# The sums over blocks of V in a fused attention kernel: loaded together, and partly added on VectorE

## The reference, cut to what matters

```python
k_sum = k.reshape(B, H, nb, block, D).max(axis=3)
v_sum = v.reshape(B, H, nb, block, D).mean(axis=3)
scores_l = where(|i - j| < 16, scale * q @ k.T, -1e9)      # a window around each position
scores_s = scale * q @ k_sum.T + log(block)                # 24 block summaries
a = softmax(concat(scores_l, scores_s))
attn = a @ concat(v, v_sum)
h = x @ w_in; solu = h * softmax(h); x = layernorm(solu) * g_ln @ w_out
out = elu(x @ w2_in) @ w2_out
```

## Time and profile before

| | |
|---|---|
| median of 3 runs | 502.55 us (502.33 to 504.12) |
| the profiled execution's own time | 502.94 us |
| its span in the profile | 501.2 us |
| granted clock, mean over the span | 0.999 |

### The profile page before, as it was taken

The page is one execution under the profiler, slowest core; times in us unless marked ns, Lnnn a source line. Parts: engine busy times, 40 slices in busy tenths (PEclk is TensorE's granted clock), DMA queues, the critical chain, the costliest instruction groups (busy, mean ns, idle before and its releaser), DMA issues.

```text
span 501.2 us, 8050 instructions
## 1 busy us (share of the span) xinstructions
PE 489.5 (98%) x3042; PEld 405.6 (81%) x3042; DVE 237.1 (47%) x634; ACT 213.5 (43%) x439; POOL 132.8 (27%) x131
## 2 busy tenths in 40 slices
PE   8889999999999999999999999999999999999997
PEld 7656666787988988999888888888888888888885
DVE  3578787278535535533655554333323323323331
ACT  3678887067525535545544343132122213212212
POOL 3995899801020020133645442000000000000000
PEclk9999999999999999999999999999999999999999
DMA  9999993700000000720000000020000002000002
GB/s 198 207 209 225 221 266 128 321 1 0 2 0 1 0 1 1 258 80 0 1 0 1 0 1 1 0 85 0 1 0 1 0 0 84 0 0 0 0 0 84
DMA packets 41669, 29.81 MB, mean 59 GB/s; under 512 B 33452, under 2 KB 35500, under 8 KB 40620
## 3 DMA queue, kind: packets, MB, share of 16 engines
q1 hardware_dynamic: 41636, 29.37, 22.8%
HBM read 26.21 MB, written 3.15 MB: 59 GB/s over the span
## 4 chain that ended last, share of the span: by engine, by line
PE 85%; DVE 5%; SPq 4%; DMA 2%; ACT 2%; issue 2%; POOL 1%; DVEq 0%
PE bank L951 12%; PE bank L953 12%; PE bank L952 12%; PE bank L1181 9%; PE bank L1179 9%; PE bank L1180 9%; PE bank L1133 4%; PE bank L1135 4%; PE bank L1134 4%; PE bank L1039 3%; PE bank L1010 2%; PE bank L960 2%; PE bank L1119 2%; DMA qraw<-in_q 2%; PE bank L1019 2%
## 5 line engine op out<-in xcount | busy, mean ns | idle before, releaser
L702 ACT ACTIVATE ex<-bank 128x512 f32<-128x512 f32 x48 | 28.7, 598 | 127.9 <-PE bank L953 127.9
L929 DVE TENSOR_SCALAR ex<-ex 128x512 f32<-128x512 f32 x48 | 21.6, 449 | 116.5 <-ACT ex L702 116.5
L953 PE MATMUL bank<-yt_lo,w2in_hi 128*128 (+1 forms) x192 | 74.8, 389 | 0.0
L952 PE MATMUL bank<-yt_hi,w2in_lo 128*128 (+1 forms) x192 | 74.8, 389 | 0.0
L1179 PE MATMUL bank<-w2out_hi,g_hi 128*128 128x512 f32 x192 | 74.8, 389 | 0.0
L1181 PE MATMUL bank<-w2out_hi,g_lo 128*128 128x512 f32 x192 | 74.7, 389 | 0.0
L951 PE MATMUL bank<-yt_hi,w2in_hi 128*128 (+1 forms) x192 | 74.7, 389 | 0.0
L1180 PE MATMUL bank<-w2out_lo,g_hi 128*128 128x512 f32 x192 | 74.7, 389 | 0.0
L934 DVE TENSOR_TENSOR g_lo<-gf,g_hi 128x512 fp32r<-128x512 f32 x48 | 46.5, 969 | 35.9 <-ACT g_hi L710 35.9
L710 ACT ACTIVATE g_hi<-gf 128x512 fp32r<-128x512 f32 x48 | 30.4, 632 | 48.9 <-DVE gf L931 48.9
L1133 PE MATMUL bank<-lnt_hi,wout_hi 128*128 128x384 f32 x128 | 45.6, 357 | 0.3 <-DVE lnt_lo L885 0.3
(11 more groups left out here) (109 smaller groups left out, 839.4 us busy)
## 6 DMA issues: line engine op xcount, KB each, us to landing
w2in_raw<-in_w_in SPq DMA_DIRECT2D x1, 4096.0 KB, 12.4
w2out_raw<-in_w_out SPq DMA_DIRECT2D x4, 1024.0 KB, 9.3
vblocks<-in_v SPq DMA_DIRECT2D x15, 256.0 KB, 6.0
kraw<-in_k SPq DMA_DIRECT2D x16, 192.0 KB, 5.9
qraw<-in_q SPq DMA_DIRECT2D x16, 192.0 KB, 4.6
out<-osb SPq DMA_DIRECT2D x12, 256.0 KB, 2.1
vw<-in_v SPq DMA_DIRECT2D x7, 384.0 KB, 7.0
win_raw<-in_w_in SPq DMA_DIRECT2D x4, 512.0 KB, 5.3
```

The lines of the kernel that those rows point to most:

```text
L952: pe.matmul(acc, al, bh, start=False, stop=False)
L953: last = pe.matmul(acc, ah, bl, start=False, stop=(i == n - 1))
```

## The change

Set 0's four block loads are issued together, straight after q0, and all of set 0 is summed at once: two levels on VectorE and three on GpSimd, each on 128 partitions. `block_means(0)` goes. Of set 1, VectorE adds the two widest levels too, at the end of its step 11 (`add_wide_levels`), and GpSimd the three narrow ones. q2 is issued ahead of set 1 instead of behind it. Pair 2's means are spread in two parts, as pair 1's were. Of the last pair's six units, VectorE now copies two instead of four (units 42 and 45), and from u = 42 on ScalarE copies the probabilities of unit u - 2 ahead of the exponentials of unit u instead of behind them.

```diff
@@ SyncE
-            load_vblocks(0, 0)
-            load_vblocks(0, 1)
+            for i in range(HPM):
+                load_vblocks(0, i)
             load_k(1)
             load_v(0)
-            load_vblocks(0, 2)
-            load_vblocks(0, 3)
             load_q(1)
             load_v(1)
             load_k(2)
+            load_q(2)
             for i in range(HPM):
                 load_vblocks(1, i)
-            load_q(2)
             load_v(2)
@@ which engine copies the turned probabilities
-            return u % 3 == 0 or u >= UNITS - T and u % 3 == 1
+            return u % 3 == 0
@@ GpSimd
-                if c < 2:
-                    pool.wait_ge(vblocks_loaded[c], 16 * (HPM if c else 2))
+                if c == 1:
+                    pool.wait_ge(wide_levels_added, 1)
...
-                rows = slice(0 if c else P // 2, P)
-                sum_blocks(vblocks[rows, c % 2, :], BLOCK * D // 2)
+                sum_blocks(vblocks[:, c % 2, :], BLOCK * D // (8 if c == 1 else 2))
...
-                if n == 1:
+                if 0 < n < PARTED:
                     spread_means(n, j0, FIRST)
                     spread_means(n, FIRST, j1)
...
             finish_v(0, FIRST, SUBS)
-            block_means(0)
             finish_v(1, 0, SUBS)
@@ ScalarE
+                copies = u >= T_LAG and u - T_LAG < UNITS and not pt_on_dve(u - T_LAG)
+                if copies and n >= PAIRS - 1:
+                    copy_pt(u - T_LAG)
                 if u < UNITS:
                     exps(u)
-                if u >= T_LAG and u - T_LAG < UNITS and not pt_on_dve(u - T_LAG):
+                if copies and n < PAIRS - 1:
                     copy_pt(u - T_LAG)
@@ VectorE
+            def add_wide_levels(c, rows, levels, loaded):
+
+                dve.wait_ge(vblocks_loaded[c], loaded)
+                x, width = vblocks[rows, c, :], BLOCK * D // 2
+                for i in range(levels):
+                    last = dve.tensor_tensor(x[:, 0:width], x[:, 0:width], x[:, width:2 * width], ALU.add)
+                    if i + 1 < levels:
+                        last.then_inc(dve_level, 1)
+                        dve.wait_ge(dve_level, i + 1)
+                    width //= 2
+                last.then_inc(wide_levels_added, 1)
+
             block_maxima(0)
             dve.wait_ge(consts_ready, 2)
-            dve.wait_ge(first_blocks_loaded, 32)
+            dve.wait_ge(vblocks_loaded[0], 16 * HPM)
             for width in (BLOCK * D // 2, BLOCK * D // 4):
-                x = vblocks[0:P // 2, 0, :]
+                x = vblocks[:, 0, :]
...
                 if t == 4 and n + 1 < PAIRS:
                     block_maxima(n + 1)
+                if u == 11:
+                    add_wide_levels(1, slice(0, P), 2, 16 * HPM)
```

More of the change, by code:

```diff
@@ L166, in fused_layers_kernel @@
         first_half_summed = sem("first_half_summed")
-        first_blocks_loaded = sem("first_blocks_loaded")
+        wide_levels_added, dve_level = sem("wide_levels_added"), sem("dve_level")
         vblocks_loaded, vsum_step, vmean_ready = [sem("vblocks_loaded0"), sem("vblocks_loaded1")], sem("vsum_step"), sem("vmean_ready")
@@ L256, in fused_layers_kernel @@
         block = ctx.enter_context(nc.Block())
-        QUAD, FIRST = P // HPM, 4
+        QUAD, FIRST, PARTED = P // HPM, 4, 3
         WIN_BEHIND = {4: (0,), 6: (1,), 7: (2, 3)}
@@ L333, in load_vblocks @@
                 if c >= 2:
-                    sp.wait_ge(vmean_ready, c)
+                    sp.wait_ge(vmean_ready, c - 1)
                 b0 = (HPM * c + i) * NB
                 b1 = min(b0 + QUAD, B * H * NB)
-                loaded = first_blocks_loaded if c == 0 and i < 2 else vblocks_loaded[c % 2]
-                sp.dma_start(vblocks[i * QUAD:i * QUAD + b1 - b0, c % 2, :], v_blocks[b0:b1, :]).then_inc(loaded, 16)
+                sp.dma_start(vblocks[i * QUAD:i * QUAD + b1 - b0, c % 2, :], v_blocks[b0:b1, :]).then_inc(vblocks_loaded[c % 2], 16)
             def load_win(i):
@@ L436, in block_means @@
             def block_means(c):
-                if c < 2:
-                    pool.wait_ge(vblocks_loaded[c], 16 * (HPM if c else 2))
-                else:
-                    pool.wait_ge(vblocks_loaded[c % 2], 16 * (HPM + (HPM if c % 2 else 2)))
-                rows = slice(0 if c else P // 2, P)
-                sum_blocks(vblocks[rows, c % 2, :], BLOCK * D // 2)
-                pool.tensor_scalar(vmean[rows, c, :], vblocks[rows, c % 2, 0:D], 1.0 / BLOCK, None, ALU.mult).then_inc(vmean_ready, 1)
-                pool.wait_ge(vmean_ready, c + 2)
+                if c == 1:
+                    pool.wait_ge(wide_levels_added, 1)
+                else:
+                    pool.wait_ge(vblocks_loaded[c % 2], 2 * 16 * HPM)
+                sum_blocks(vblocks[:, c % 2, :], BLOCK * D // (8 if c == 1 else 2))
+                pool.tensor_scalar(vmean[:, c, :], vblocks[:, c % 2, 0:D], 1.0 / BLOCK, None, ALU.mult).then_inc(vmean_ready, 1)
+                pool.wait_ge(vmean_ready, c + 1)
             def first_means():
                 pool.wait_ge(first_half_summed, 1)
-                rows = slice(0, P // 2)
-                sum_blocks(vblocks[rows, 0, :], BLOCK * D // 8)
-                pool.tensor_scalar(vmean[rows, 0, :], vblocks[rows, 0, 0:D], 1.0 / BLOCK, None, ALU.mult).then_inc(vmean_ready, 1)
+                sum_blocks(vblocks[:, 0, :], BLOCK * D // 8)
+                pool.tensor_scalar(vmean[:, 0, :], vblocks[:, 0, 0:D], 1.0 / BLOCK, None, ALU.mult).then_inc(vmean_ready, 1)
                 pool.wait_ge(vmean_ready, 1)
@@ L496, in finish_v @@
                 fill_halo(n, max(j0, 1), j1)
-                if n == 1:
+                if 0 < n < PARTED:
                     spread_means(n, j0, FIRST)
                     spread_means(n, FIRST, j1)
-                if n > 1:
+                if n >= PARTED:
                     spread_means(n, j0, j1)
@@ L1027, in attend @@
                     pe.wait_ge(halo_filled, n + 2 if n else 1)
-                    pe.wait_ge(means_spread, 2 * n + 6 if n > 1 else 4 * n + 2)
+                    pe.wait_ge(means_spread, 2 * n + 2 * PARTED + 2 if n >= PARTED else 4 * n + 2)
                 if n == 0 and 2 * t == FIRST:
                     pe.wait_ge(halo_filled, 2)
-                if n < 2 and 2 * t == FIRST:
+                if n < PARTED and 2 * t == FIRST:
                     pe.wait_ge(means_spread, 4 * n + 4)
```

## The result

| | before | after |
|---|---|---|
| median of 20 runs each | 502.88 us (501.96 to 504.68) | 504.85 us (502.69 to 508.26) |
| ratio after to before | | 1.0036, 95% interval 1.0022 to 1.0050 |
| the profiled execution's own time, span | 502.94, 501.2 us | 507.55, 505.7 us |
| runs with a mean granted clock of 0.998 or more | | 7 of 20, median 503.6 us |

The change costs 0.36%, which is inside what I called no change, and 1.85 us above the 503.0 that I named. The times of after fall into steps with the mean granted clock of each run: 502.7 to 504.2 us at 0.999 or 1.0 (7 runs), 504.5 to 505.0 at 0.996 or 0.997 (4), 505.1 to 505.5 at 0.993 (3), 506.7 to 508.3 at 0.990 or 0.987 (6). The profiled execution of after is one at 0.990.

The account below looks back on a forecast made before the run. TensorE, busy for 98% of the span, was taken as the bound, so its waits count. Terms +1.0 - 1.3 + 1.9 - 1.2 = +0.4 us gave 503.3 for the profiled execution, 503.0 as median; range 501.0 to 505.5.

Parts of the forecast that it names:

- the class: Whole kernel: time within 0.5% of before, 500.04 to 505.06 us, chance 0.80; faster 0.07, slower 0.13.
- clock rival: Front: TensorE idles from about 12.5 to 14.5 us and its clock falls, +2.5 us, time 505.5; chance 0.12.
- The two cases named as leaving the class: Absorbed additions with early blocks, 500.1 us (faster, 0.07); late blocks with no last-pair gain, 505.0 (slower, with the clock, 0.13).
- signs of being right: Additions start at 11 to 12.5 us; no q1, q2 or last-pair waits; 1.5 to 2 us idle before prep_k(3); rows_product +0.4.
- sign of being wrong: No idle at prep_k(3); additions over 2.5 us; longer front matmuls; attend waiting on the spread means in pair 2.
- Step 1: Front: first additions wait for four blocks, not two, starting at 11.6 us; net +1.0 us (+0.6 to +1.8).
- the other anchor: Front: the old fourth block's lead, about 0.7 MB, puts the landing of set 0's last block at 12.4 us.
- Step 2: q2 ahead of set 1: q2 lands near 23.5 us and TensorE's whole 1.32 us wait goes, -1.3 us.
- Step 3: Two additions in VectorE's step 11 delay low_x and so prep_k(3), +1.9 us (near 0 to 3.9).
- VectorE absorbed nothing: Rival at VectorE's step 11: VectorE absorbs the additions, the sum loses 1.9, time 501.1 us; chance 0.17.
- GpSimd was in time for pair 2: Near-tie at pair 2's first means: GpSimd needs 4.5 us, TensorE comes after 4.9; hidden by 0.4 us.
- Step 4: Last pair: both TensorE waits on ScalarE's copies, 0.56 and 0.65 us, go; -1.2 us (-1.3 to +0.3).

Follow-up runs that it names:

- c: The kernel before with the last pair's edits alone (VectorE copies units 42 and 45, ScalarE's copy ahead of the exponentials): median 502.45 us, ratio 0.9985.
- i: g with 5 throwaway identity products on TensorE ahead of its wait for q1: median 502.00 us, ratio 0.9973 to the kernel before.
- a: The changed kernel with set 1 summed wholly on GpSimd again, no additions in VectorE's step 11: median 502.51 us, ratio 0.9985 to the kernel before.
- b: The changed kernel with 12 throwaway identity products on TensorE ahead of prep_k(3): median 504.59 us, ratio 1.0031 to the kernel before.
- e: The changed kernel with 6 throwaway identity products on TensorE ahead of prep_k(3): median 504.47 us, ratio 1.0011 to the kernel before.
- f: The kernel before with only set 0's four block loads together and all of set 0 summed at once: median 502.84 us, ratio 0.9988.
- d: The kernel before with only q2's two loads moved ahead of set 1's four: median 503.34 us, ratio 1.0006.
- k: e with 9 instead of 6 identity products at the front, so both gaps are partly filled: median 502.96 us, ratio 0.9992 to the kernel before.
- g: The kernel before with q2 ahead of set 1, pair 2's means spread in two parts and the last pair's edits: median 501.87 us, ratio 0.9967.
- h: a with VectorE's scores of units 0 and 1 ahead of its first additions: median 502.83 us, ratio 0.9991 to the kernel before.

## Why the prediction was right, and where not

**The range and the class held, in part by luck.** The time lay inside 501.0 to 505.5 and within 0.5% of before. The named 503.0 was worked out for a clock that holds; the full-clock median is 503.6, and the median of all runs a mixture, at +1.97 us over before where the sum had +0.4. It stayed under 505.06, the edge of no change, by 0.2 us, and the range reached so far only for a clock rival that was priced at another place. The two cases named as leaving the class, 500.1 and 505.0, both lie inside its bounds of 500.04 and 505.06; that is a slip in the chances.

**The signs.** Of the signs of being right, all held but the last: `rows_product` came 4.57 us later and not 0.4. One sign of being wrong showed too, matmuls at the front longer than before: the first 24 of K (pair 0), at 5.24 us, took 2.62 us, and 1.66 in the profile before. That is not the change, since they took 2.03 in c and 2.61 in i, whose front loads are the old ones, and VectorE's wait for the blocks covered it.

**Step 1, at the high side of its range.** The additions started at 12.27 in the profile of after and at 11.28 to 11.79 in those of a, b, e and f; I took 11.6, with 12.4 by the other anchor. The addition on 128 partitions took 1.95 us, as taken from GpSimd's rows. `prep_q(1)` came 1.56 us later in after and 0.6 to 0.8 in a, b and f; the term was +1.0 with the range 0.6 to 1.8.

**Step 2, right in the trace.** The wait for q2 is gone, worth 1.29 us against 1.32. But it is one term with step 1 and not a second one: f shows that the old wait would have hidden most of step 1's loss, and d that q2's move by itself brings 0.2 us at full clock, of 1.3. Why so little in d isn't settled. The sum priced q2's place and left out what GpSimd's means then cost; the rows of d put that at about 0.9 us at full clock, an estimate.

**Step 3, right to 0.1 us.** The forecast was +1.9 with `low_x` as the releaser; the trace has a wait of 1.91 and a shift of 1.86. VectorE absorbed nothing, though it is busy for only about 8 of 10 us: in the profile of after it has no idle piece between 29 and 35.6 us, and the next ones lie behind the order that `prep_k(3)` waits for. GpSimd was in time for pair 2, in k at full clock too.

**Step 4, right in the trace.** Both waits gone, 1.46 us in after and 1.20 in c against 1.2; at the end of the run c shows 0.6 to 0.9 of it.

**What failed: the clock rival, in its place and price.** I gave it 0.12, at the front, with 2.5 us. A lower clock is real in 13 of 20 runs, and the larger part, in the profile and by b and e, is at the gap of step 3, which the prediction described ("TensorE idles 1.5 to 2 us before `prep_k(3)`") without asking what the clock does there. In the profile it cost 3.90 us, twice the gap itself; at the front, about 1.3. I leaned on the longest idle of one trace, 1.32 us with the clock held. That trace was one of the good draws: 28 of 97 runs of the kernel before beside the experiments lose 1.4 to 1.9 us, most likely to the same thing at the wait for q1. The Trainium skill, "TensorE: Matmul & The Clock Gate", section "HAM oscillation — how this bites in real kernels", names a longer idle gap than any here. The traces differ: 1.91 us and 1.67 us were enough in some runs. The measurement decides; what the Trainium skill gives there is no safe distance.

## What to carry to other kernels

An engine that is busy for 80% of a stage has no room for a piece of 2 us if its next small result is waited for at once; price such a piece at its full length, and then ask what the waiting TensorE's clock will do. Where TensorE idles for 1.5 to 2 us, as here, the loss comes in two sizes that differ from run to run, so one profile isn't enough: read the granted clock of every run, compare full-clock runs for the mechanism and medians for the verdict. Idle waits that can't be removed can be filled with throwaway products, but only up to the wait's length.

## What was not expected of the hardware

- The granted clock fell after idle stretches of only 1.58 us (e), 1.67 us (d), 1.91 us (after) and 2.01 us (g), but not in every run: the kernel before held it through 0.99 and 1.32 us, and h through 2.09 us. It then read 0.50 for some 3 us (d, e and g) to 10 us (after) while TensorE worked without a break.
- At the lower level the same six matmuls of `prep_k` took 1.51 us instead of 0.85, and the stage lost 3.90 us over about 10 us of low clock.
- At the very start the granted clock says nothing of this. It reads 1.00 from 5 to 7 us in the profiles of before and after, while the same 24 matmuls took 1.66 and 2.62 us, and 1.53 in d.
